# Accumulator banks of a pairwise feed-forward stage, and a split interleaved with additions, in a fused fp32 kernel

## What is computed

```python
# attention, 8 heads of 64: a causal window of 96 keys and 8 global keys, with a distance bias
a = softmax(where(keep, q @ k.T / 8 - slope * dist, -1e9));  x = a @ v
# mixing over tokens (rank 32), then a feed-forward layer 512 -> 2048 -> 512
u = x + ((x.transpose(0, 2, 1) @ U) @ V).transpose(0, 2, 1)
y = u + maximum(u @ w_ch1, 0) @ w_ch2
# gated spatial layer, 512 -> 2 * 512 -> 512
h = maximum(y @ w_in, 0);  u2, v2 = h[..., :512], h[..., 512:]
v_n = (v2 - mean(v2)) / sqrt(var(v2) + 1e-6)
out = (u2 * (einsum('ts,bsd->btd', w_spatial, v_n) + b)) @ w_out
```

## Time and profile before

| | |
|---|---|
| median of 3 runs | 510.71 us |
| the profiled execution | 510.94 us |
| its span, first to last instruction | 508.9 us |
| TensorE busy | 98% of the span |
| VectorE busy | 56% |
| ScalarE busy | 42% |
| GpSimd busy | 41% |
| mean granted TensorE clock | 1.000 |

### The profile page before, as it was taken

How to read it: one execution, slowest core, us unless ns; L and a number is a source line. 1 busy time by engine, 2 the same in 40 slices (tenths; PEclk the granted TensorE clock), 3 DMA queues, 4 the chain that set the end, 5 groups by cost and what they waited for, 6 DMA issues and landing times.

```text
span 508.9 us, 7827 instructions
## 1 busy us (share of the span) xinstructions
PE 499.4 (98%) x2822; PEld 413.3 (81%) x2822; DVE 285.7 (56%) x666; ACT 214.6 (42%) x490; POOL 208.8 (41%) x178
## 2 busy tenths in 40 slices
PE   8999999999999999999999999999999999999997
PEld 7788577787888888778787787887788998889995
DVE  5887688521269456465564565648687345530530
ACT  7988678532235633232341222414654113331121
POOL 6796656353336666753565635423430000000000
PEclk9999999999999999999999999999999999999999
DMA  8810800123123422112222021031500000110002
GB/s 237 291 53 25 310 2 2 44 83 101 67 88 109 134 82 82 41 45 82 82 84 82 1 82 55 19 103 32 176 1 1 1 0 22 41 52 12 1 21 104
DMA packets 14552, 36.28 MB, mean 71 GB/s; under 512 B 2480, under 2 KB 2480, under 8 KB 14512
## 3 DMA queue, kind: packets, MB, share of 16 engines
q1 hardware_dynamic: 12640, 32.35, 18.9%
q10 hardware_dynamic: 1872, 3.41, 1.8%
HBM read 32.61 MB, written 3.15 MB: 70 GB/s over the span
## 4 chain that ended last, share of the span: by engine, by line
PE 86%; DVE 8%; ACT 3%; issue 1%; DMA 1%; ACTq 0%; SPq 0%; DVEq 0%
PE bank L1209 29%; PE bank L1481 15%; PE bank L1416 9%; PE bank L1338 9%; PE bank L1499 7%; PE bank L1506 5%; DVE uT L772 4%; PE bank L1262 4%; PE bank L1244 3%; PE bank L1229 3%; ACT prob L941 2%; PE bank L1280 1%; DVE y_split L777 1%; PE bank L1285 1%; DMA qk_raw<-in_qk 1%
## 5 line engine op out<-in xcount | busy, mean ns | idle before, releaser
L458 POOL TENSOR_TENSOR w_slot<-stage,w_slot 128x1024 fp32r<-128x1024 f32 x30 | 73.1, 2447 | 65.7 <-ACT w_slot L1007 65.7
L772 DVE TENSOR_TENSOR uT<-bank,uT 128x512 f32<-128x512 f32 x68 | 46.0, 690 | 28.2 <-PE bank L1506 26.1
L941 ACT ACTIVATE prob<-prob,row_min 128x256 f32<-128x256 f32 (+1 forms) x96 | 46.1, 483 | 13.5 <-DVE row_min L593 13.5
L1209 PE MATMUL bank<-sp_slot,vn 128*128 128x384 f32 x288 | 50.3, 334 | 0.0
L1209 PEld LDWEIGHTS bank<-sp_slot,vn 128*128 128x128 f32 x288 | 50.0, 188 | 0.2
L1499 PE MATMUL bank<-hid,w_slot 128*128 128x512 f32 x192 | 48.5, 395 | 0.8
L1481 PE MATMUL bank<-u_op,s_slot 128*128 128x512 f32 x192 | 47.6, 389 | 0.0
L1416 PE MATMUL bank<-hid,w_slot 128*128 128x512 f32 x192 | 47.0, 393 | 0.0
L1338 PE MATMUL bank<-u_split,w_slot 128*128 128x512 f32 x192 | 46.4, 391 | 0.0
L1506 PE MATMUL bank<-hid,w_slot 128*128 128x512 f32 x192 | 46.1, 389 | 0.0
L1499 PEld LDWEIGHTS bank<-hid,w_slot 128*128 128x128 f32 x192 | 35.4, 188 | 11.3 <-DVE uT L772 4.0
(11 more groups left out here) (121 smaller groups left out, 824.2 us busy)
## 6 DMA issues: line engine op xcount, KB each, us to landing
stage<-in_w_ch SPq DMA_DIRECT2D x32, 512.0 KB, 3.3
qk_raw<-in_qk SPq DMA_DIRECT2D x23, 256.0 KB, 4.7
v_all<-in_v SPq DMA_DIRECT2D x12, 256.0 KB, 4.9
out_dram<-o_stage ACTq DMA_DIRECT2D x12, 256.0 KB, 2.0
stage<-in_w_spT SPq DMA_DIRECT2D x6, 384.0 KB, 3.1
stage<-in_w_in SPq DMA_DIRECT2D x4, 512.0 KB, 3.4
stage<-in_w_out SPq DMA_DIRECT2D x2, 512.0 KB, 3.5
V_raw<-in_V SPq DMA_DIRECT2D x4, 96.0 KB, 4.6
```

Of the source, the lines that this page charges most:

```text
L458: nc.gpsimd.tensor_tensor(dst[:, LO, :], stage[n % 2][:, 0:w], dst[:, HI, :].bitcast(F32), ALU.subtract).then_inc(w_lo, 1)
L772: vec.tensor_tensor(y, c_bank[k][:], y, ALU.add).then_inc(y_sum, 1)
L941: last = sc.activation(prob[r][:, e, 0:w], prob[r][:, e, 0:w], ACT.Exp, bias=row_min[:, k:k + 1], scale=-1.0, accum_out=row_sum[:, q:q + 1])
L1209: last = mm(out_ap, lhs(a), rhs(c), start=(n == 0), stop=(n == 3 * len(terms) - 1))
```

## The change

Three edits, none of which adds or removes a matmul, an addition or a split.

The sums of the third chunk are accumulated in `seven_bank` in place of `c_bank` (`y_bank`). So the third chunk's first four matmuls wait no more for `y_sum`, but for the additions that read banks 4 and 5 (`part_sum`). In the next pair each product of `seven` that starts a bank waits for that bank's sum, and the second chunk's first matmuls wait for sums of the pair before.

`g_ring` begins with banks 0 to 3, and the first eight items wait for one sum each, where items four to seven had waited for all sums.

In the last pair VectorE makes a low half of the first chunk after each sum of the second chunk. Every `v` item waits for y's low half and for `w_in`'s row block by row block.

```diff
-        g_ring = [bank[i] for i in (6, 7, 4, 5, 0, 1, 2, 3)]
+        g_ring = [bank[i] for i in (0, 1, 2, 3, 6, 7, 4, 5)]
...
+        def y_bank(e):
+            return (c_bank if e < KD or (e - KD) // KD % 2 == 0 else seven_bank)[e % KD]
...
-                vec.tensor_tensor(y, c_bank[k][:], y, ALU.add).then_inc(y_sum, 1)
+                vec.tensor_tensor(y, y_bank(e)[:], y, ALU.add).then_inc(y_sum, 1)
...
                 for x in range(2 * KD):
-                    if i == PAIRS - 1 and x == KD:
-                        for k in range(KD):
-                            split_y(k)
                     sum_y(KD + 2 * KD * i + x)
+                    if i == PAIRS - 1 and x < KD:
+                        split_y(x)
...
                     if i == 0:
                         pe.wait_ge(u_lo, KD + 2 * op + 2)
+                    elif not more:
+                        pe.wait_ge(y_sum, KD + 2 * KD * (i - 1) + KD + held + 1)
...
                             if a == HI and m == HI:
-                                pe.wait_ge(y_sum, 2 * KD * i + KD * n + k + 1)
-                            mm(c_bank[k][:], w[r][:, a, 512 + k * P:512 + (k + 1) * P], hid2[r][n][:, m, :],
+                                if n == 0:
+                                    pe.wait_ge(y_sum, max(0, 2 * KD * i - KD) + k + 1)
+                                elif k >= 2:
+                                    pe.wait_ge(part_sum, 5 * i + k + 2)
+                            mm(y_bank(e + k)[:], w[r][:, a, 512 + k * P:512 + (k + 1) * P], hid2[r][n][:, m, :],
...
-                if 4 <= n < NB:
-                    pe.wait_ge(y_sum, KD + 2 * KD * PAIRS)
+                if n < NB:
+                    pe.wait_ge(y_sum, 2 * KD * PAIRS - KD + n + 1)
...
-                    pe.wait_ge(y_lo, KD * (c + 1))
-                    pe.wait_ge(w_lo, load_no("in", 3) + 1)
-                    last = product(dst[:], [
-                        (lambda a, k=k: y_split[c][:, a, k, r * P:(r + 1) * P],
-                         lambda m, k=k: in_slot[k][:, m, FH:2 * FH]) for k in range(KD)])
+                    for k in range(KD):
+                        pe.wait_ge(y_lo, KD * c + k + 1)
+                        pe.wait_ge(w_lo, load_no("in", k) + 1)
+                        for p, (a, m) in enumerate(PASSES):
+                            last = mm(dst[:], y_split[c][:, a, k, r * P:(r + 1) * P], in_slot[k][:, m, FH:2 * FH],
+                                      start=(k == 0 and p == 0), stop=(k == KD - 1 and p == 2))
```

More of the change, by code:

```diff
@@ L1488, in contract_pair @@
                 for n in range(2):
+                    e = KD + 2 * KD * i + KD * n
                     r = n
@@ L1505, in contract_pair @@
                         for a, m in PASSES:
-                            last = mm(c_bank[k][:], w[r][:, a, 512 + k * P:512 + (k + 1) * P], hid2[r][n][:, m, :],
-                                      start=False, stop=(a == LO), skip_group_check=True)
+                            last = mm(y_bank(e + k)[:], w[r][:, a, 512 + k * P:512 + (k + 1) * P],
+                                      hid2[r][n][:, m, :], start=False, stop=(a == LO), skip_group_check=True)
                         last.then_inc(pair_acc, 1)
```

## The result

The changed kernel takes **506.93 us** (median of 6 runs, 506.8 to 507.0); the kernel before, measured beside it, 510.76 us. The ratio is 0.992, with a 95% interval of 0.9907 to 0.9933. Forecast were 506.9 us, in a range of 506.1 to 508.4 us. The profiled execution took 506.97 us with a span of 505.0 us, 3.9 us shorter than before.

A forecast was written before the change was run, and what follows sets the result against it. TensorE's stream, busy 499.4 of 508.9 us, was taken as the bound. Gains of 3.20 + 0.62 = 3.82 us brought 510.94 to 507.12 us, less 0.23 us for the median: 506.9 us, range 506.1 to 508.4 us.

The forecast's parts named there:

- The size of a gap: TensorE's wait for VectorE's sums in `contract_pair`: 0.40 us lost per pair, read from starts, eight times, 3.20 us.
- the idle loads: Upper bound of the gain, taking each idle weight load in full: 4.0 + 0.7 = 4.7 us, 506.0 us.
- The turn between pairs: Next pair's seven products wait for third-chunk sums on the new banks: 0.9 us left in hand, cost 0.
- the slower rival: Next pair's first product waits for all third-chunk sums, seven times: 514.7 or 517.4 us, chance 0.04.
- the milder form: The slower rival with TensorE restarting 1.1 us late in seven turns: 7.8 us, 514.7 us.
- The stricter form: The slower rival with sums that don't come earlier, 1.5 us late in seven turns: 10.5 us, 517.4 us.
- The first item: First item after the last pair, with low halves interleaved and awaited row by row: 0.62 us removed.
- the second part: Low halves between sums and the first item started bank by bank and row by row: 0.62 us removed.
- the lower of my own bounds: Least gain, if the first item gains nothing: 3.20 us, 507.5 us.
- The added waits: 88 more waits on TensorE, taken at 0 each; upper end 0.04 us each.
- What follows behind: Stream after the first item up to the first spatial product: cost 0, 0.1 us in hand there, 0.4 us before TensorE.

The follow-up runs named there:

- e6: Changed kernel, but in the next pair each product that starts a bank waits for all four third-chunk sums: 514.93 us.
- e7: Changed kernel with one more VectorE addition ahead of the third chunk's first sum, in seven pairs: 507.32 us.
- e8: Changed kernel with two more VectorE additions ahead of the third chunk's first sum, in seven pairs: 511.84 us.
- e1: Kernel before with only the banks changed; low halves stay where they stood and v items wait at their head for all of them: 508.14 us.
- e3: Changed kernel without the waits by row: each v item waits at its head for all four low halves and row blocks: 508.02 us.
- e4: Changed kernel without the interleaving: low halves between the sums of the second and third chunk, waits by row kept: 506.92 us.
- e2: Kernel before with the interleaving and the waits by row, but banks 0 to 3 for both chunks: 517.26 us.
- e11: Changed kernel with the items' banks in the old order (6, 7, 4, 5, 0 to 3), the first four waiting for third-chunk sums: 508.59 us.
- e10: As e6, but with the wait for the sums ahead of the waits for the weights: 514.74 us.

## Why the prediction was right

**The size of a gap.** "The loss is 0.40 us per pair, not the 0.50 us of idle weight load": the pair went from 20.79 to 20.40 us, and 506.9 us was forecast, 506.93 us measured. An agreement within 0.03 us is in part chance, since the levels of the sets differ by some 0.15 us. With the idle loads it would have been 506.0 us. The difference of 0.1 us per pair fits loads that run ahead (by 353.66 - 353.43 = 0.23 us in the stream), and e6 has it too: its loads idle 1.27 us at a turn, and the stream loses 1.14 us.

**The turn between pairs.** The 0.9 us in hand are there (0.93 us in the trace) and are real: one addition of 0.69 us fits into them, but for the one turn in which VectorE idled besides; two don't. "At 1.1 us, 7.8 us, 514.7 us" was the price of the slower rival in the milder form; built, it took 514.93 us. The stricter form (1.5 us, 517.4 us) was too dear, since the sums do come earlier with the matmuls. "It begins to cost from 0.9 us of delay" holds as well. The sum that was waited for ended 1.15 us (e7, first turn), 1.53 us (e8) and 2.74 - 0.69 = 2.05 us (e6) late, the stream lost 0.27, 0.65 and 1.14 us, and 0.88, 0.88 and 0.91 us were hidden.

**The first item.** The laid-out ends of the low halves, 353.87, 356.13 and 357.45 us, moved by the 2.84 us by which this pass comes earlier, are 351.03, 353.29 and 354.61 us; the trace has 351.01, 353.27 and 354.47 us. What failed is the split into parts. "Removed: 8 waits of 0.40 us = 3.20 us. All of it lies on the path" holds only with the second part beside it: e1 shows seven. So the lower of my own bounds, "3.20 us if the first item gains nothing (507.5 us)", was wrong, and 508.14 us was measured. The low halves end when VectorE and GpSimd are through, so a TensorE that is 0.40 us faster waits 0.40 us longer. And I credited the interleaving and the waits by row together; e3 and e4 show that the rows bring all of it. The total is right all the same, because both parts were in the kernel and the sum counts each gap once. I had the times to see this: low half 0 would have been ready at 353.87 us without interleaving, well ahead of the load that asks for it.

**The added waits.** Cost 0, as forecast, now with 192 more of them.

**What follows behind.** The timeline ahead of the first spatial product, as the earlier trace rows:

```profile
388.97 0.55 DVE L862 TENSOR_SCALAR v_raw<-v_raw,mean_var,rstd 128x512 f32<-128x512 f32 x1 [0.43 <-issue]
...
389.71 0.62 ACT L1136 ACTIVATE vn<-v_raw 128x512 fp32r<-128x512 f32 x1
390.37 0.69 DVE L867 TENSOR_TENSOR vn<-v_raw,vn 128x512 fp32r<-128x512 f32 x1 [0.85 <-ACT vn L1136]
391.51 4.60 PEld L1212 LDWEIGHTS bank<-sp_slot,vn 128*128 128x128 f32 x26
```

390.37 + 0.69 = 391.06 us against 391.51 us: 0.45 us in hand, 0.4 us forecast. The normalised v is ready at 388.97 + 0.55 = 389.52 us, 0.19 us before ScalarE reads it, with 0.1 us forecast. The load comes 3.86 us earlier than at 395.37 us, the whole gain.

## What to carry to other kernels

Measure a stall by the distance between starts of the busy stream, not by the idle time of the engine that runs ahead. A gain can be counted for each place only if the next thing that is waited for moves with it; an end set by other engines (here four low halves held by GpSimd) gives the last stretch back. When a wait for several pieces starts a long run, waiting piece by piece can be worth more than making the pieces earlier, and where accumulators change banks, the banks of what follows have to change with them (1.7 us here).

## What was not expected of the hardware

**The clock.** After 2.79 and 1.72 us of idle time with one matmul between them (e2), TensorE ran at a granted clock of 0.50 for the next 4 us, and some 2.3 us were lost on top of what the waits cost; all four executions had a mean granted clock of 0.993. One gap between matmuls of 1.3 us (e11) left the mean at 1.000, seven gaps of 0.8 to 0.9 us (e6, e10) at 0.999, which is no more than the kernel before shows between its executions (0.999 and 1.000). The Trainium skill, page "TensorE: Matmul & The Clock Gate", section "Part 1: The HAM clock gate", has the same two levels.

**Two waits on one matmul.** The load was released 0.10 to 0.11 us after the sum's end with the sums' wait written behind the weights' (e6: 233.37 to 233.47 us; e8: 232.65 to 232.76 us), and 0.04 us after it with the wait written ahead (e10). Why only half of the 0.06 us reaches the stream stays open.
